# Attention and two feed-forward layers on one core: three instead of two scores ahead of the first value product of each half head

## The chip, the cores and the metric

The kernel runs on one core of a Trainium2 chip. The metric is the device time of one execution in microseconds (us); the median of several executions is compared.

## The reference, cut to what matters

Inputs are q, k, v of shape (2, 8, 768, 64) in fp32, a projection of 64 x 6, and the weights of two feed-forward layers. 16 heads of 768 tokens are worked on.

```python
q_bits = (q @ proj) > 0                      # 6 bits per token, likewise k_bits
mask = bucket(q_bits)[:, None] == bucket(k_bits)[None, :]
scores = where(mask, q @ k.T / 8, -1e9)
attn = exp(scores - max(scores)); attn = attn / (sum(attn) + 1e-9)
x = attn @ v                                 # per head, heads side by side: (1536, 512)
h = maximum(maximum(x @ w1, x @ w2), x @ w3) # 512 -> 768
y = h @ w_out                                # 768 -> 512
out = elu(y @ w_in) @ w_out2                 # 512 -> 2048 -> 512
```

## The kernel before, in words

**Precision.** Each fp32 operand of TensorE is split in a high and a low part of type fp32r, and a product is three matmuls (high x high, high x low, low x high). The mask is worked into the scores' matmuls as further rows of the operands, so one score is two matmuls (L621, L622).

**Slots.** Attention is a software pipeline over slots, one for each head, with some ahead of the first and behind the last (`all_slots`, L102; slots 4 to 11 are a loop of two turns with four slots each). Every engine runs its own list of work for a slot, ordered by hand and tied to the others by counting semaphores. A slot has 12 steps (`STEPS`), and `LAG` is 6: a half is 6 steps. In the slot of head h, TensorE does

- the 12 scores of head h (`scores`, L612), one a step: a tile of 128 keys by 384 queries; steps 0 to 5 are the first half of the queries, 6 to 11 the second. They go in turn to three PSUM banks (`RING` is 3), so score n waits until ScalarE has taken the exponentials of score n - 3 (`exp_done`, L618);
- 12 maxima of head h+1 (`maxima`, L597; L609), in the steps that `MAX_AT` (L65) sets: numbers 0 and 1 in step 0, 2 in step 1, 3 and 4 in step 2, 5 in step 3, 6 in step 4, 7 and 8 in step 5, 9 and 10 in step 6, 11 in step 7. They alternate between two PSUM banks, and maximum n waits until VectorE has reduced maximum n - 2 (`mx_read`, L607);
- 12 value products (`weigh`, L625; L636 to L638), six steps behind the scores: in steps 0 to 5 those of the second half of head h-1, in steps 6 to 11 those of the first half of head h. Six of them add up in one bank, `pv_ps`, there being only this one; the sixth is followed by L645, which signals `pv_ready`. The first of each six waits (`o_read`, L631) until ScalarE has copied the bank away;
- in odd slots transposes of q and k (L580) in steps 0 and 6, in even slots hash projections (L592 to L594) in steps 3 and 6. The last of these is in slot 12; slots 13 to 15 have none, and slot 15, the last head, has no maxima either;
- in step 8 the turn: the transpose of the row maxima (L667), which waits for `max_done` (L666), and a column sum (L672).

ScalarE in each step takes two exponentials of a score, `probs` (L378) and `p_hi` (L379). In steps 0 and 6 it first copies the finished `pv_ps` away, x (L356) and inv (L357) (`outcome`, L349). It also rounds v (`v_hi`, L387) behind the exponentials of step 0, and has work in steps 1, 3, 4 and 7 (L365, L418, L412).

VectorE reduces the maxima (L492). Between the reductions of maxima 2 and 3 it makes `v_lo` (L479), after maximum 11 the row maxima (L496). POOL makes `p_lo` (L335), one for each step, and one xl for each slot from 3 on (L341). SP moves operands.

**Order on TensorE** (`emit`, L648). In step 0 or 6 it is: the score of that step, the maxima, transposes or projections, the score of the next step, and then the first value product of the new half. In step 1 or 7: maxima, value product. In step 2 or 8: score, maxima, value product.

Behind attention TensorE goes through the feed-forward layers (`three`, L703, and L1050 to L1054).

Of the kernel before, what the change touches and what calls it, by code (L numbers as in the profile page):

```python
# [58 lines left out]
LAG = T  # L59
# [58 lines left out]
def wait(eng, sem, count):  # L118

    if not isinstance(count, int) or count > 0:  # L120
        eng.wait_ge(sem, count)


def attention(nc, q, k, v, proj, w1, w2, w3, xh, xl, raw, wh, wl, banks, w_loaded, w_split, w_ready, f_ready):
    ctx = ExitStack()
    with ctx:  # L126
# [436 lines left out]
        def _(pe):  # L563
            pe.wait_ge(consts, 3)

            def transposes(s, x, n):

                src = q_raw if x == "q" else k_raw
                par = (s.off + 3) // 2 % 2
                if n == 1:  # L570
                    pe.wait_ge(q_in[par], s.count(8, 56 - 16 * par))

                    wait(pe, bits_done, s.count(1, 3))
                else:
                    pe.wait_ge(k_in[par], s.count(8, 56 - 16 * par))
                    if s.off > FIRST_SLOT:
                        pe.wait_ge(lo_done, s.count(1, 4))
                out = turned[x, s.off == FIRST_SLOT]
                for t in range(T):
                    last = pe.transpose(out[:, t // TH, (t % TH) * P:(t % TH + 1) * P],  # L580
                                        src[:, par, t, :, :].rearrange("p a d -> p (a d)"), ident[:])
                last.then_inc(t_ready, 1)

            def project(s, x, n):


                pe.wait_ge(lo_done, s.count(1, 2 + n if s.off == FIRST_SLOT + 1 else 4))
                if s.off == FIRST_SLOT + 1:
                    pe.wait_ge(proj_split, 2)
                x_bank = misc[:, n - 1, 0:HALF]  # L590
                for c in range(2):
                    pe.matmul(x_bank, proj_hi[:, c, :], lo[x][:, c, :], start=(c == 0), stop=False)  # L592
                    pe.matmul(x_bank, proj_lo[:, c, :], hi[x][:, c, :], start=False, stop=False)
                    last = pe.matmul(x_bank, proj_hi[:, c, :], hi[x][:, c, :], start=False, stop=(c == 1))  # L594
                last.then_inc(hash_ready, 1)

            def maxima(s, n):  # L597

                m = s.off + 1
                if n == 0:  # L600

                    pe.wait_ge(spread1[m % 2], s.count(SPREAD1 / 2, SPREAD1 * (1.5 if m % 2 == 0 else 1)))
                    if m == 0:
                        pe.wait_ge(consts, 11)
                    wait(pe, mrow_done, s.count(1, 1))

                wait(pe, mx_read, s.count(STEPS, STEPS + n - 1))  # L607
                t, half = n // 2, (n % 2) * HALF
                pe.matmul(mx_ps[n % 2][:, 0:HALF], operands[m % GROUP][0:96, Q1, t * P:(t + 1) * P],  # L609
                          operands[m % GROUP][0:96, K1, half:half + HALF], start=True, stop=True).then_inc(mx_ready, 1)  # L610

            def scores(s, step):  # L612
                head = operands[s.off % GROUP]
                if step == 0:
                    pe.wait_ge(spread2[s.off % 2], s.count(SPREAD2 / 2, SPREAD2 / (1 if s.off % 2 == 0 else 2)))
                    pe.wait_ge(mrow_done, s.count(1, 1))

                wait(pe, exp_done, s.count(STEPS, step - RING + 1))  # L618
                t, half = step % T, step // T * HALF
                out = st_ps[step % RING][:, 0:HALF]  # L620
                pe.matmul(out, head[:, K1, t * P:(t + 1) * P], head[:, Q1, half:half + HALF], start=True, stop=False)  # L621
                pe.matmul(out, head[:, K2, t * P:(t + 1) * P], head[:, Q2, half:half + HALF], start=False, stop=True  # L622
                          ).then_inc(st_ready, 1)

            def weigh(s, step):  # L625

                h = s.off - (1 if step < LAG else 0)
                kt, at = step % T, (step - LAG) % STEPS
                if kt == 0:

                    wait(pe, o_read, s.count(4, -2 if step < LAG else 0))  # L631
                    if step == LAG:
                        pe.wait_ge(vl_done, s.count(1, 1))
                pe.wait_ge(pl_done, s.count(STEPS, step - LAG + 1))
                out, kept = pv_ps[:, 0:HALF], (STEPS * s.off + step - LAG) % KEPT
                pe.matmul(out, v_hi[:, h % 2, kt, :], p_hi[:, kept, :], start=(kt == 0), stop=False)  # L636
                pe.matmul(out, v_hi[:, h % 2, kt, :], p_lo[:, kept, :], start=False, stop=False)  # L637
                pe.matmul(pv_ps[0:D, 0:HALF], v_lo[:, h % 2, kt, :], p_hi[:, kept, :], start=False, stop=False  # L638
                          ).then_inc(pv_step, 1)
                if kt == T - 1:  # L640
                    if step > LAG:
                        pe.wait_ge(total_done, s.count(2, 2))
                        pe.wait_ge(empty_done, s.count(1, 1))
                    half = at // T * HALF
                    pe.matmul(out, total[:, h % 2, :], empty[:, h % 2, half:half + HALF], start=False, stop=True  # L645
                              ).then_inc(pv_ready, 1)

            def emit(s):  # L648
                for step in range(STEPS):
                    if s.has_st and step % LAG != 1:  # L650
                        scores(s, step)
                    if s.has_max:
                        for n in range(MAX_BEFORE[step], MAX_BEFORE[step + 1]):
                            maxima(s, n)
                    for i, x in enumerate("qk"):
                        if s.has_tp and step == TP_AT[i]:
                            transposes(s, x, i + 1)
                        if s.has_hash and step == HASH_AT[i]:
                            project(s, x, i + 1)
                    if s.has_st and step % LAG == 0:  # L660

                        scores(s, step + 1)
                    if s.has_half1 if step < LAG else s.has_half0:
                        weigh(s, step)
                    if step == TURN_AT and s.has_max:
                        pe.wait_ge(max_done, s.count(1, 2))  # L666
                        pe.transpose(mt_all, row_max[:, (s.off + 1) % 2, :], ident[:]).then_inc(mt_ready, 1)  # L667
                    if step == TURN_AT and s.has_st:
                        pe.wait_ge(vsum_done, s.count(1, 1))
                        if s.off == 0:  # L670
                            pe.wait_ge(consts, 15)
                        pe.matmul(sum_all, ones[:], val_sum[:], start=True, stop=True).then_inc(sum_ready, 1)  # L672
                if s.off == HEADS:


                    pe.wait_ge(w_ready, 1)
                    pe.wait_ge(xl_done, HEADS // B)
                    pe.wait_ge(exp_done, HEADS * STEPS)
                    for u, x in EARLY:
                        if (u, x) == (1, 0):  # L680
                            pe.wait_ge(w_ready, 2)
                            pe.wait_ge(mrow_done, HEADS)
                            pe.wait_ge(total_done, 2 * HEADS)
                        expert(pe, banks, wh, wl, xh, xl, u, x, f_ready)

            all_slots(pe, emit)


# [36 lines left out]
def expert(pe, banks, wh, wl, xh, xl, u, x, f_ready):  # L725

    m, c = UNIT_ORDER[u]
    pairs = []
    for t in range(KD):
        w = slice(x * DM + t * P, x * DM + (t + 1) * P)  # L730
        pairs.append(((wh[:, m % 2, w], wl[:, m % 2, w]), (x_tokens(xh, t, c), x_tokens(xl, t, c))))
    three(pe, banks[:, EXPERTS * (u % 2) + x, :], pairs).then_inc(f_ready, 1)
# [376 lines left out]
```

## Time and profile before

| | |
|---|---|
| three runs | 751.24, 752.99, 754.25 us; median 752.99 |
| the profiled execution, its own time | 751.45 us |
| its span, first to last instruction | 749.7 us |
| mean granted TensorE clock | 0.984 of 2.4 GHz |
| TensorE matmul busy | 719.0 us, 96% |
| VectorE, ScalarE, POOL busy | 379.8, 420.2, 366.5 us (51, 56, 49%) |

PE is TensorE's matmul row, PEld its weight load, DVE is VectorE, ACT ScalarE, POOL GpSimd. L-numbers are lines of the kernel. In a timeline a row has start, duration, engine, line, operation, output<-inputs, shape and count, and in brackets the idle time of the engine just before and what ended it. Matmuls overlap in their rows, since the shown duration has the way through the array in it; their rate is read from the starts. Attention takes about the first 287 us of the span.

### The profile page before, as it was taken

The numbers are of one execution on the slowest core, as the hardware profiler recorded it, in microseconds if no ns is written. First come the engines' busy times: TensorE is split into PE (matmuls) and PEld (weight loads), VectorE is DVE, ScalarE is ACT, GpSimd is POOL, SyncE is SP. The second block draws the span as 40 slices with busy tenths as digits, with TensorE's granted clock in tenths as the row PEclk, the third lists the DMA queues.
The fourth block names the chain that finished last, engine by engine and source line by source line (L and its number), as shares of the span: only waits on it lengthen the run. The fifth ranks groups of instructions, "written<-read, shape, count | busy, mean of one in ns | idle before, by whom it ended". The sixth has DMA issues, their size and how long they took to land.

```text
span 749.7 us, 10429 instructions
## 1 busy us (share of the span) xinstructions
PE 719.0 (96%) x3440; PEld 615.9 (82%) x3440; DVE 379.8 (51%) x612; ACT 420.2 (56%) x818; POOL 366.5 (49%) x332
## 2 busy tenths in 40 slices
PE   4699999999999989999999999999999999999998
PEld 3489999999999877788888888878888888888886
DVE  3677988889888854322222221144334343444333
ACT  1288989999898983222221121255556555555553
POOL 5077888888888883011110011154444545444452
PEclk9599999999999999999999999999999999999999
DMA  6766364563626100211000001033335332343331
GB/s 133 167 145 149 85 137 99 133 144 81 144 62 142 49 1 0 85 43 42 23 1 20 22 21 43 29 113 104 94 96 156 89 109 86 110 143 100 97 99 56
DMA packets 79629, 64.70 MB, mean 86 GB/s; under 512 B 29152, under 2 KB 68832, under 8 KB 79584
## 3 DMA queue, kind: packets, MB, share of 16 engines
q1 hardware_dynamic: 79584, 64.12, 33.6%
q8 instruction: 25, 0.41, 0.2%
q14 instruction: 20, 0.16, 0.1%
HBM read 40.91 MB, written 3.15 MB: 59 GB/s over the span
## 4 chain that ended last, share of the span: by engine, by line
PE 59%; DVE 0%; ACT 0%; issue 0%
PE banks L707 14%; PE banks L708 14%; PE banks L709 14%; PE banks L1050 6%; PE banks L1054 6%; PE banks L1051 6%; DVE g_sb L993 0%; DVE g_sb L989 0%; DVE out_sb L963 0%; ACT gh L948 0%; ACT neg L943 0%
## 5 line engine op out<-in xcount | busy, mean ns | idle before, releaser
L860 POOL TENSOR_TENSOR wl<-raw,wh 128x512 fp32r<-128x512 f32 (+2 forms) x104 | 143.4, 1398 | 301.7 <-ACT wh L876 301.7
L335 POOL TENSOR_TENSOR p_lo<-probs,p_hi 128x384 fp32r<-128x384 f32 x192 | 196.4, 1041 | 64.0 <-ACT p_hi L379 63.2
L707 PE MATMUL banks<-xh,wh 128*128 128x512 f32 x408 | 158.9, 390 | 0.5 <-PEq L126 0.5
L708 PE MATMUL banks<-xl,wh 128*128 128x512 f32 x408 | 158.7, 389 | 0.0
L709 PE MATMUL banks<-xh,wl 128*128 128x512 f32 x408 | 158.7, 389 | 0.0
L492 DVE TENSOR_REDUCE half_max<-banks 128x1 f32<-128x384 f32 x192 | 99.7, 547 | 28.2 <-PE banks L609 27.4
L378 ACT ACTIVATE probs<-banks 128x384 f32<-128x384 f32 x192 | 95.1, 495 | 23.2 <-PE banks L622 19.1
L379 ACT ACTIVATE p_hi<-banks 128x384 fp32r<-128x384 f32 x192 | 95.2, 496 | 0.0
L989 DVE TENSOR_SCALAR g_sb<-banks 128x512 f32<-128x512 f32 x48 | 33.2, 692 | 119.8 <-ACT neg L943 119.8
L707 PEld LDWEIGHTS banks<-xh,wh 128*128 128x128 f32 x408 | 76.6, 188 | 17.1 <-issue 0.9
L709 PEld LDWEIGHTS banks<-xh,wl 128*128 128x128 f32 x408 | 76.6, 188 | 15.9
L708 PEld LDWEIGHTS banks<-xl,wh 128*128 128x128 f32 x408 | 76.6, 188 | 15.7
L1050 PE MATMUL banks<-wh,gh 128*128 128x512 f32 x192 | 74.9, 390 | 0.2 <-ACT gh L948 0.2
L1054 PE MATMUL banks<-wh,gl 128*128 128x512 f32 x192 | 74.9, 390 | 0.0
L1051 PE MATMUL banks<-wl,gh 128*128 128x512 f32 x192 | 74.7, 389 | 0.0
L636 PE MATMUL banks<-p_hi,v_hi 128*128 128x384 f32 x192 | 67.0, 349 | 8.0 <-ACT inv L357 7.7
L943 ACT ACTIVATE neg<-banks 128x512 f32<-128x512 f32 x48 | 28.7, 598 | 68.1 <-PE banks L709 68.1
L876 ACT ACTIVATE wh<-raw 128x512 fp32r<-128x512 f32 (+2 forms) x104 | 64.7, 665 | 2.6 <-PE banks L1054 0.3
L638 PE MATMUL banks<-p_hi,v_lo 128*64 128x384 f32 x192 | 65.1, 339 | 0.0
L637 PE MATMUL banks<-p_lo,v_hi 128*128 128x384 f32 x192 | 64.4, 335 | 0.0
L922 ACT ACTIVATE hh<-e 128x512 fp32r<-128x512 f32 x18 | 11.4, 632 | 92.4 <-DVE e L973 92.4
L948 ACT ACTIVATE gh<-g_sb 128x512 fp32r<-128x512 f32 x48 | 30.4, 633 | 40.8 <-DVE g_sb L993 40.8
(108 smaller groups left out, 1175.9 us busy)
## 6 DMA issues: line engine op xcount, KB each, us to landing
operands<-wh SPq DMA_DIRECT2D x36, 384.0 KB, 6.9
raw<-in_moe_w_in SPq DMA_DIRECT2D x48, 256.0 KB, 2.7
raw<-in_moe_w_out SPq DMA_DIRECT2D x48, 256.0 KB, 2.8
wl<-wh SPq DMA_DIRECT2D x12, 384.0 KB, 5.8
raw<-in_moe_w SPq DMA_DIRECT2D x18, 256.0 KB, 3.8
q_raw<-in_q SPq DMA_DIRECT2D x16, 192.0 KB, 3.6
k_raw<-in_k SPq DMA_DIRECT2D x16, 192.0 KB, 3.8
v_raw<-in_v SPq DMA_DIRECT2D x16, 192.0 KB, 2.4
```

The lines of the kernel that those rows point to most:

```text
L335: pool.tensor_tensor(p_lo[:, at, :], probs[:, step % RING, :], p_hi[:, at, :].bitcast(FP32), ALU.subtract).then_inc(pl_done, 1)
L378: act.activation(probs[:, step % RING, :], scores, ACT.Exp, scale=SCALE)
L379: act.activation(p_hi[:, (STEPS * s.off + step) % KEPT, :], scores, ACT.Exp, scale=SCALE).then_inc(exp_done, 1)
L492: dve.tensor_reduce(half_max[:, m % 2, n // 2, n % 2:n % 2 + 1], mx_ps[n % 2][:, 0:HALF], AX.X, ALU.max).then_inc(mx_read, 1)
L636: pe.matmul(out, v_hi[:, h % 2, kt, :], p_hi[:, kept, :], start=(kt == 0), stop=False)
L707: pe.matmul(out, sh, mh, start=first, stop=False)
L708: pe.matmul(out, sh, ml, start=False, stop=False)
L709: last = pe.matmul(out, sl, mh, start=False, stop=final)
L860: pool.tensor_tensor(wl[:, j, at:at + cols], raw[:, j, at:at + cols], wh[:, j, at:at + cols].bitcast(FP32), ALU.subtract).then_inc(w_ready, 1)
L1050: pe.matmul(acc[t], gh[:, n % 2, cols], w2h, start=(k == 0), stop=False)
L1051: pe.matmul(acc[t], gh[:, n % 2, cols], w2l, start=False, stop=False)
L1054: last = pe.matmul(acc[t], gl[:, n % 2, cols], w2h, start=False, stop=(k == M2 - 1))
```

## The change

On entering each half, TensorE issues the score of step 2 (or 8) right behind that of step 1 (or 7), ahead of the first value product of the half, and not any more at the start of step 2 (or 8). The matmuls, their operands, banks and waits stay the same.

```diff
             def emit(s):
                 for step in range(STEPS):
-                    if s.has_st and step % LAG != 1:
+                    if s.has_st and step % LAG not in (1, 2):
                         scores(s, step)
                     if s.has_max:
                         for n in range(MAX_BEFORE[step], MAX_BEFORE[step + 1]):
                             maxima(s, n)
...
                     if s.has_st and step % LAG == 0:

                         scores(s, step + 1)
+                        scores(s, step + 2)
                     if s.has_half1 if step < LAG else s.has_half0:
                         weigh(s, step)
```

## Rows read from the trace of the kernel before

**Rows 1.** The page, part 1: busy us, share of the span, instructions.

```profile
PE 719.0 (96%) x3440; PEld 615.9 (82%) x3440; DVE 379.8 (51%) x612; ACT 420.2 (56%) x818; POOL 366.5 (49%) x332
```

**Rows 2.** Waits on PE; idle time before L636: us, times, longest.

```profile
PE banks L636 <- ACT inv L357: 7.7, 13, 2.1
...
  ACT inv L357: 20.3, 30
```

**Rows 3.** Timeline, first half of an even slot: PE, its loads, DVE.

```profile
158.54 0.34 PE L622 MATMUL banks<-wl 128*128 128x384 f32 x1
...
159.19 0.44 PE L636 MATMUL banks<-p_hi,v_hi 128*128 128x384 f32 x1 [0.31 <-ACT inv L357]
...
159.82 0.34 PE L609 MATMUL banks<-operands 96*128 96x384 f32 x1
...
160.20 0.56 DVE L492 TENSOR_REDUCE half_max<-banks 128x1 f32<-128x384 f32 x1 [0.34 <-PE banks L609]
...
160.67 0.79 DVE L479 TENSOR_TENSOR v_lo<-v_raw,v_hi 128x384 fp32r<-128x384 f32 x1
...
161.38 1.01 DVE L492 TENSOR_REDUCE half_max<-banks 128x1 f32<-128x384 f32 x2
...
161.75 0.19 PEld L622 LDWEIGHTS banks<-wl 128*128 128x128 f32 x1
...
161.98 0.19 PEld L609 LDWEIGHTS banks<-operands 96*128 96x128 f32 x1
162.10 0.34 PE L609 MATMUL banks<-operands 96*128 96x384 f32 x1
```

**Rows 4.** Timeline, first half of an odd slot: PE, DVE, POOL.

```profile
144.88 0.34 PE L609 MATMUL banks<-wl 96*128 96x384 f32 x1
...
145.26 0.56 DVE L492 TENSOR_REDUCE half_max<-banks 128x1 f32<-128x384 f32 x1 [0.56 <-PE banks L609]
...
145.73 0.59 DVE L479 TENSOR_TENSOR v_lo<-v_raw,v_hi 128x384 fp32r<-128x384 f32 x1
...
146.19 1.02 POOL L335 TENSOR_TENSOR p_lo<-probs,p_hi 128x384 fp32r<-128x384 f32 x1 [0.28 <-ACT p_hi L379]
...
146.32 1.02 DVE L492 TENSOR_REDUCE half_max<-banks 128x1 f32<-128x384 f32 x2
```

**Rows 5.** Timeline, second half of the same odd slot: PE, DVE, PEld.

```profile
151.94 0.33 PE L622 MATMUL banks<-operands 128*128 128x384 f32 x1
152.30 0.44 PE L636 MATMUL banks<-p_hi,v_hi 128*128 128x384 f32 x1
152.58 0.34 PE L637 MATMUL banks<-p_lo,v_hi 128*128 128x384 f32 x1
...
152.93 0.34 PE L609 MATMUL banks<-wl 96*128 96x384 f32 x1
...
153.91 0.18 DVE L496 TENSOR_REDUCE row_max<-half_max 128x12 f32<-128x24 f32 x1
...
154.35 0.14 PEld L667 LDWEIGHTS banks<-ident,row_max 128*128 128x128 f32 x1
```

**Rows 6.** Timeline, slot 0: v_lo on DVE and p_lo on POOL.

```profile
37.19 1.36 DVE L479 TENSOR_TENSOR v_lo<-v_raw,v_hi 128x384 fp32r<-128x384 f32 x1
...
37.13 1.00 POOL L335 TENSOR_TENSOR p_lo<-probs,p_hi 128x384 fp32r<-128x384 f32 x1 [0.28 <-ACT p_hi L379]
```

**Rows 7.** Timeline of slot 13, and busy times of one stretch of slot 15.

```profile
244.92 0.44 PE L636 MATMUL banks<-p_hi,v_hi 128*128 128x384 f32 x1 [0.68 <-ACT inv L357]
...
240.10 0.49 ACT L378 ACTIVATE probs<-banks 128x384 f32<-128x384 f32 x1 [0.29 <-PE banks L622]
...
271.00:276.00 5.00, 2.25 (x10) 1.25 (x10) 0.50 (x1) 4.90 (x11) 3.91 (x4) 1.00 0.00 0
```

**Rows 8.** Busy times of 277 to 281 us: PE, PEld, DVE, ACT, POOL, then granted clock.

```profile
277.00:281.00 4.00, 4.00 (x16) 3.81 (x16) 2.22 (x4) 2.05 (x6) 2.99 (x4) 0.57 0.00 0
```

## The prediction

> **What bounds the kernel now.** I read the page first: TensorE is busy 96% of the span [rows 1], so time can only come from its few pauses or from doing less work, and the change does the same matmuls in another order. The page's chain of waits runs through the feed-forward part, which the diff does not touch; the diff acts in attention. So the waits came next: the value product's first matmul (L636) waits for the second evacuation of its single accumulator (L357) 7.7 us in all on the matmul row, and the idle time before it, with the weight load's row counted too, is 20.3 us at 30 places [rows 2]. These overlap, so neither is the price. I took the price from starts in the timeline. Back-to-back matmuls of 384 columns start 0.175 us apart (152.58 to 152.93 holds two) [rows 5].
>
> Entry of an even slot, where nothing else stands between the scores: last score matmul at 158.54, value product at 159.19, so 0.65 - 0.175 = 0.475 us lost [rows 3]. Entry of the second half of an odd slot, where transposes fill part of it: 151.94 to 152.30, 0.185 us lost, and 0.28 instead of 0.175 to the next matmul, another 0.10 [rows 5]. In the steady part (slots 1 to 12) there are six of each kind. Odd slots at step 0 and even slots at step 6 have transposes or projections there and lose nothing. In slots 13 to 15 there are six more, of which the one at 244.92 (0.68 idle) stands here [rows 7].
>
> **The change, part by part.** One score, two matmuls, 2 x 0.175 = 0.35 us, moves from behind the second value product to ahead of the first. It has no transfer, and passes no work of SP's or POOL's queue. It does pass the maxima of step 1 (maximum 2 in the first half, 11 in the second) and two value products. Its own wait is for the previous exponentials (step 5's for step 8). The outcome's two copies follow that exponential on ScalarE, so the score's wait is over about 1 us before that of the value product queued behind it: price 0.
>
> What matters is what becomes close together. Between maximum 2 and maxima 3 to 5 there stood this score; maximum n may start only when VectorE has read n-2.
>
> *A. First half of even slots, six.* The value product cannot start before the copy, so maximum 2 stays at 159.82. VectorE reads it from 160.20, then makes v_lo (160.67, 0.79 us), then reads maxima 3 and 4 from 161.38, the first by about 161.93 (0.56 us). Maximum 5's weight load starts at 161.98, though its predecessor's started at 161.75 and loads follow 0.175 apart: it is already late by 0.05, waiting for that read [rows 3]. So this chain (copy, value product, maximum 2, v_lo, maximum 3, maximum 5) is closed before the change; filling the pause at its start cannot bring maximum 5 at 162.10 forward. The freed 0.35 us turns up as a wait at maxima 4 and 5. Gain 0; bounds -0.35 and +0.1 each (-2.1, +0.6).
>
> *B. First half of odd slots, six.* No pause there, so value product and maximum 2 go 0.35 later: 144.88 becomes 145.23. VectorE reads maximum 2 0.38 us after its start for 0.56 us [rows 4]; with the 0.05 that a release takes in [rows 3], maximum 4's load may start 0.99 after maximum 2 and its matmul 0.12 later (161.98 to 162.10), 1.11 in all. TensorE would be there after 0.88 (one maximum, three products, one maximum: five of 0.175). That adds 0.23. v_lo starts at 146.08, and maximum 3 is then read in time for maximum 5. Cost 0.22 x 6 = +1.3 us; bounds 0 and the whole score, 0.35 x 6 = +2.1.
>
> *C. Second half of odd slots, six.* The 0.185 + 0.10 of pause goes, since 0.35 more work stands ahead: 0.28 x 6 = -1.7 us; bounds -2.1 and 0.
>
> *D. The turn of the row maxima, slots 0 to 14.* In the second half the score leaves the stretch between maximum 11 (152.93) and the turn's transpose (L667), whose load is at 154.35 [rows 5]. Row maxima are ready at 153.91 + 0.18 = 154.09, 1.16 after maximum 11; released at 1.21, the matmul starts at 1.33. Without the score TensorE is there after 0.175 + 6 x 0.175 = 1.23. A new wait of 0.10 x 15 = +1.5 us; bounds 0 and 0.2 x 15 = +3.0.
>
> *E. Slots 13 to 15.* The first-half entries of 13 and 14 are closed by the chain of A, but step 3's score still comes 0.12 earlier, and ScalarE was idle 0.29 waiting for it [rows 7], so the next copy comes 0.12 earlier too. Their second halves have no v_lo and long pauses: 0.35 each. Slot 15 has no maxima, but ScalarE is back to back there (busy 4.90 of 5.00 us [rows 7]); only the score left behind its second entry gains, 0.35. Sum -(0.12 + 0.35) x 2 - 0.35 = -1.3 us; bounds -2.1 and 0.
>
> *F. Slot 0.* It enters no half with the accumulator in use. Maximum 2 is later, but v_lo ends when POOL is done anyway [rows 6]: 0; bounds 0 and +0.5.
>
> Sum: 0 + 1.3 - 1.7 + 1.5 - 1.3 + 0 = -0.2 us. The profiled execution took 751.45, so its like would take 751.25; it lay 1.54 below the median of the runs, 752.99, against which I state the forecast: **752.8 us**.
>
> Here the trace and the notes can be weighed. Both [rows 3] and [rows 5] show the weight load starting no earlier than the release, and the matmul some 0.1 behind its usual place. The Trainium skill (TensorE: Matmul & The Clock Gate, Architectural detail) says that TensorE's queue can pull weight loads ahead of matmuls in flight. If that reached past a semaphore wait, B would cost about 0.11 and D nothing, and the sum would be about -2.4. The rows do not show it, so the sum keeps the 0.1.
>
> **Rivals.** *Full gain:* the maxima's reads are quick enough after all, and every pause shrinks by up to 0.35: 6 x 0.28 + 12 x 0.35 = 5.9, so 747.1 us. For it: the pauses are there. Against it: the late load of maximum 5 in [rows 3]. Chance 0.10.
>
> *Slower, v_lo behind POOL:* in slot 0 v_lo started at 37.19, 0.06 after a p_lo of POOL, and took 1.36 instead of 0.59, ending 0.42 after POOL did [rows 4, 6]. In odd slots v_lo moves to 146.08, and the next p_lo starts at 146.19 [rows 4]. The margin is 0.11. If v_lo comes second it ends at 147.21 + 0.42 = 147.63, maximum 3 is read by 148.1, and maximum 5's matmul starts near 148.3 instead of 147.20: +1.1 in place of 0.22, 6 x 0.88 = +5.3, so 758.1 us. It decides where v_lo slips by more than 0.11 us. Chance 0.12. The Trainium skill (SBUF — State Buffer, Who interferes with whom) has a rule for it: a VectorE instruction with two inputs in SBUF contends with a GpSimd instruction that reads SBUF, and the first gets the shared port for its whole length. By that rule, the trace agrees, with the 1.36.
>
> *The clock:* from 277 to 281 us the granted clock averages 0.57, so mostly 1.2 instead of 2.4 GHz, after a stretch with TensorE busy 2.25 of 5.00 us [rows 8, 7]. A score now stands inside that pause. If the drop goes, some ten matmuls save 0.14 each (384 columns at 1.2 GHz are 0.32 us, against 0.175): 1.4 us, 751.4 us. Chance 0.08; still no change by the bound below.
>
> **How the numbers follow.** About 0.5%, 3.8 us, is what a measurement can tell from no change: below 749.2 faster, above 756.8 slower. My sum keeps 0.70. Its bounds are not independent; with B and D at their low ends it is -3.0 (750.0), with both high +2.1 (755.1), and runs spread 1.5 around their median. The range 749.5 to 756.0 holds this case and the clock's; full gain and the POOL case are left out. Faster: 0.10 plus a little for A opening, 0.12. Slower: 0.12 plus 0.01, 0.13. Same: 0.75.
>
> **What would show it.** In the changed trace the pause ahead of L636 should be below 0.2 at even entries and gone in odd second halves; L609 should gain waits for L492, about 0.2 at maximum 4 in every first half, and maximum 5 in even slots should again start 2.28 after maximum 2; L667 should wait about 0.1 for L496. An even slot's first half, from value product to maximum 5, keeps its 2.91 us. Wrong if the wait at L636 shrinks and no wait at L609 takes its place (full gain), or if v_lo in odd slots takes over 1 us (slower).

## The result and the profile after

The changed kernel took 756.54 us (median of five runs, 756.35 to 757.35). The kernel before, beside it on the same chip, took 752.92 (five runs, 751.24 to 754.25). The ratio is 1.0065, with a 95% interval of 1.0049 to 1.0080: **slower by about 0.65%**, just outside the range of 749.5 to 756.0. The ratio is not the quotient of these two medians, which is 1.0048: the median of before and three of its five runs lie in a cluster near 753, and against the 751.6 that later groups of runs of the same kernel gave (below) it is 1.0066. The profiled execution of the changed kernel is one of 756.84 us with a span of 755.0, 5.39 and 5.3 above those of before, so the two traces hold the whole difference and some more.

The page after (its part 1, and from part 5 the group of the value product's first matmul):

```profile
PE 724.0 (96%) x3440; PEld 614.0 (81%) x3440; DVE 381.2 (50%) x612; ACT 419.1 (56%) x818; POOL 367.5 (49%) x332
...
L636 PE MATMUL banks<-p_hi,v_hi 128*128 128x384 f32 x192 | 66.8, 348 | 2.3 <-ACT inv L357 2.2
```

The instruction counts are those of [rows 1]. TensorE's busy time has grown by 5.0 us with the same work, so it can't tell where time was lost: a matmul row grows when the clock is lower. The waits in attention, from 50 to 290 us of the kernel after, say more (engine, line, what it waited for: us, times, longest):

```profile
ACT probs L378 <- PE banks L622: 21.4, 22, 2.1
PEld banks L609 <- DVE half_max L492: 11.6, 27, 1.0
...
PEld banks L636 <- ACT inv L357: 5.1, 10, 1.7
PE banks L609 <- DVE half_max L492: 3.8, 8, 0.7
...
PEld banks L668 <- DVE row_max L496: 2.7, 14, 0.2
...
PE banks L636 <- ACT inv L357: 2.2, 4, 1.4
```

The wait that the change aims at did shrink, from 7.7 us at 13 places [rows 2] to 2.2 at 4. In its place the maxima (L609) wait for VectorE, 3.8 us on the matmul row and 11.6 on that of the loads (the two overlap). And ScalarE waits 21.4 us for scores; in the same window of the kernel before it was 12.6.

To find where, I took the starts of L645, the last matmul of each half, and their distances. Each row stands for the halves of that kind; in us:

| half | before | after | difference in all |
|---|---|---|---|
| odd slots 1, 3, 7, 9, 11, first half | 7.71 to 7.75 | 7.88 to 7.90 | +0.83 |
| slot 5, first half | 7.70 | 8.76 | +1.06 |
| odd slots, second half, six | 7.16 to 7.32 | 6.98 to 6.99 | -1.61 |
| even slots 2 and 4, first half | 8.71, 8.72 | 8.72, 8.72 | 0.0 |
| **even slots 6, 8, 10, 12, first half** | 8.62 to 8.65 | 9.94 to 9.97 | **+5.26** |
| even slots, second half, six | 7.28 to 7.34 | 7.33 to 7.39 | +0.27 |
| slots 13, 14, first halves | 7.52, 7.66 | 7.51, 7.66 | 0.0 |
| slots 13, 14, second halves; 15, first | 7.23, 7.37, 6.23 | 6.87, 7.01, 5.87 | -1.08 |
| slot 15, second half | 10.76 | 11.67 | +0.91 |

The first L645 comes 0.26 earlier than before and the last one 5.38 later, at 292.40 against 287.02. Nearly all of the loss is in four halves. Slot 8's shows how, in the timeline of the kernel after (it answers to [rows 3]; rows of TensorE, its loads, VectorE, ScalarE and POOL):

```profile
160.35 1.01 POOL L335 TENSOR_TENSOR p_lo<-probs,p_hi 128x384 fp32r<-128x384 f32 x1
...
160.41 1.38 DVE L535 TENSOR_TENSOR x<-x,inv 128x384 f32<-128x384 f32 x1
...
160.91 0.44 PE L636 MATMUL banks<-p_hi,v_hi 128*128 128x384 f32 x1
...
161.70 1.64 DVE L492 TENSOR_REDUCE half_max<-banks 128x1 f32<-128x384 f32 x3
...
162.30 0.44 PE L609 MATMUL banks<-operands 96*128 96x384 f32 x1 [0.60 <-DVE half_max L492]
...
163.07 2.29 POOL L335 TENSOR_TENSOR p_lo<-probs,p_hi 128x384 fp32r<-128x384 f32 x2 [0.31 <-ACT p_hi L379]
...
163.25 1.24 DVE L479 TENSOR_TENSOR v_lo<-v_raw,v_hi 128x384 fp32r<-128x384 f32 x1
...
164.75 0.49 ACT L378 ACTIVATE probs<-banks 128x384 f32<-128x384 f32 x1 [1.00 <-PE banks L622]
...
165.02 0.44 PE L609 MATMUL banks<-operands 96*128 96x384 f32 x1 [0.31 <-DVE half_max L492]
```

The same place in the kernel before, rows that the prediction did not use:

```profile
158.38 1.41 POOL L335 TENSOR_TENSOR p_lo<-probs,p_hi 128x384 fp32r<-128x384 f32 x1
...
158.39 0.54 DVE L535 TENSOR_TENSOR x<-x,inv 128x384 f32<-128x384 f32 x1
```

Read L535 first. It is VectorE's division of a finished head (`divide`, x times inv), the last thing in its list for a slot, from slot 2 on, and so the one of an odd slot stands ahead of maximum 0 of the even slot. The description of the kernel before leaves it out. Both its inputs are in SBUF. Before, it started 0.01 us after a p_lo of POOL and took 0.54, while that p_lo took 1.41 in place of 1.01. After, it started 0.06 behind a p_lo and took 1.38, ending 0.43 after POOL. So of the two, one keeps its time and the other ends late, and the change has turned round who comes first. The 0.84 lost there make the reductions of maxima 0 to 2 late (161.70), maximum 2 waits 0.60 on the matmul row, v_lo starts at 163.25, 0.18 behind a p_lo (163.07), and takes 1.24; before it came 0.64 behind one (160.03) and took 0.79 [rows 3], maximum 5 comes 2.72 after maximum 2 instead of 2.28, and ScalarE, without scores for 1.00 us, hands the delay on.

The starts of the division and of that p_lo in four of the five pairs of the steady part, both kernels:

| end of slot | before: division, p_lo | after: division, p_lo | division took, before, after |
|---|---|---|---|
| 3 | 96.44, 96.45 | 96.38, 96.38 | 0.56, 0.56 |
| 5 | 127.42, 127.45 | 128.20, 128.02 | 0.56, 1.25 |
| 7 | 158.39, 158.38 | 160.41, 160.35 | 0.54, 1.38 |
| 9 | 189.33, 189.34 | 192.57, 192.52 | 0.54, 1.38 |

The end of slot 11 is like that of 9 (224.80, 1.37). Slot 4, which follows the one tie that was still won, keeps its 8.72, and slot 2 has no division ahead of it. A lost tie is not dear everywhere: at the ends of the even slots 4 to 10 the division came second in the kernel before as well (1.23 to 1.26), and run 2 below, which frees it there, leaves the odd first halves at 7.69 to 7.85, against 7.70 to 7.75.

Why it tips, at the end of slot 7: both engines are back to back up to this point, on chains that start at different matmuls. VectorE's starts at the reduction of maximum 11, 5.08 us ahead of the division before and 5.05 after (153.31 to 158.39, 155.36 to 160.41). POOL's starts at the p_lo of step 8, three p_lo ahead of the one in the tie (155.46 before, 157.42 after). The change issues the score of step 8 earlier and thereby maximum 11 later against it: from the reduction to that p_lo it was 2.15 us, and is now 2.06. These 0.09 are more than the margin.

The stretch that answers to [rows 4], the first half of odd slot 7 after:

```profile
147.08 0.34 PE L609 MATMUL banks<-wl 96*128 96x384 f32 x1
...
147.45 0.56 DVE L492 TENSOR_REDUCE half_max<-banks 128x1 f32<-128x384 f32 x1 [0.92 <-PE banks L609]
147.93 0.55 DVE L479 TENSOR_TENSOR v_lo<-v_raw,v_hi 128x384 fp32r<-128x384 f32 x1
...
148.04 1.31 POOL L335 TENSOR_TENSOR p_lo<-probs,p_hi 128x384 fp32r<-128x384 f32 x1 [0.29 <-ACT p_hi L379]
...
148.06 0.19 PEld L609 LDWEIGHTS banks<-wl 96*128 96x128 f32 x1 [0.27 <-DVE half_max L492]
```

v_lo stays 0.11 ahead of POOL and takes 0.55 us; in four of the other odd slots it is 0.11 to 0.19 ahead, with the same 0.55. Its second half (it answers to [rows 5]):

```profile
154.99 0.34 PE L609 MATMUL banks<-wl 96*128 96x384 f32 x1
...
155.95 0.18 DVE L496 TENSOR_REDUCE row_max<-half_max 128x12 f32<-128x24 f32 x1
...
156.03 0.34 PE L638 MATMUL banks<-p_hi,v_lo 128*64 128x384 f32 x1
...
156.18 0.14 PEld L668 LDWEIGHTS banks<-ident,row_max 128*128 128x128 f32 x1 [0.19 <-DVE row_max L496]
...
156.20 0.31 PE L668 MATMUL banks<-ident,row_max 128*128 128x128 f32 x1
```

The load of the turn waits 0.19, but the matmul starts 0.17 after the one before it: no pause.

### The profile page after: what moved, and what is told of

It reads as the page before. It is cut to its first block, busy times and chain, and to the rows that moved or that the text cites. A ratio compares the mean times of both kernels' runs of the same rounds, so it can differ in the third digit from the quotient of the medians.

```text
span 755.0 us, 10429 instructions
## 1 busy us (share of the span) xinstructions
PE 724.0 (96%) x3440; PEld 614.0 (81%) x3440; DVE 381.2 (50%) x612; ACT 419.1 (56%) x818; POOL 367.5 (49%) x332
## 4 chain that ended last, share of the span: by engine, by line
PE 59%; DVE 0%; ACT 0%; issue 0%
PE banks L708 14%; PE banks L709 14%; PE banks L710 14%; PE banks L1051 6%; PE banks L1055 6%; PE banks L1052 6%; DVE g_sb L994 0%; DVE g_sb L990 0%; DVE out_sb L964 0%; ACT gh L949 0%; ACT neg L944 0%
## 5 line engine op out<-in xcount | busy, mean ns | idle before, releaser
L636 PE MATMUL banks<-p_hi,v_hi 128*128 128x384 f32 x192 | 66.8, 348 | 2.3 <-ACT inv L357 2.2
L621 PE MATMUL banks<-operands 128*128 128x384 f32 x144 | 51.8, 360 | 2.3 <-ACT p_hi L379 2.3
```

## The experiments

My theory: the loss is the tie at L535, some 1.3 us for each of the four that are lost, with little else changed. The rival: the even first halves lose through the entry itself (three scores ahead, maximum 2 late, v_lo late), whatever the division does. Each kernel is compared with the kernel before of its own group of runs, whose medians were 751.55 (runs 1 to 4), 751.74 (5, 8, 9 and 10), 751.57 (6, 11 and 12) and 751.60 (7). The ratios are estimated from the single runs and need not be the quotients of the medians. In the expectations the runs go by labels: e1 to e5 are runs 1 to 5, e6, e7 and e8 are 8, 9 and 10, e9 is 6, e10 and e11 are 11 and 12, and e12 is 7.

**1. The change, with the division moved.** The tie goes, the change stays.

```diff
@@ VectorE, emit
+                    if n == 2 and s.has_split:
+                        divide(Slot(s.off - 1, s.g))
@@ end of the slot
-                if s.has_unit:
-                    divide(s)
```

> Three scores ahead as in the change, but VectorE's division (L535, two SBUF inputs) is issued behind the second reduction of the next slot instead of ahead of the first. Theory 'lost port': in slots 6, 8, 10 and 12 of the changed kernel the division starts 0.05 to 0.2 us after a p_lo of POOL, takes 1.25 to 1.38 instead of 0.55 us, and delays maxima 2 to 5; with it out of the way these four first halves fall from 9.95 to about 8.7 us, so about 756.5 - 5.2 = 751.3 us. Rival 'chain of maxima': the tighter order of maxima 2 to 5 alone makes the 9.95, the division is only late with them; then 756.5 stays.

Measured: 751.14 us (749.18 to 752.61, ten runs), 0.9991 of before [0.9974, 1.0007]. The four halves are back at 8.63 to 8.66, those of slots 2 and 4 stay at 8.71 and 8.74. The tile x on VectorE, and the division in slot 8:

```profile
L535 DVE TENSOR_TENSOR x<-x,inv x16: 545/549/1371, 81.8 to 291.2; 128x384 f32<-128x384 f32 x16
...
158.97 0.55 DVE L535 TENSOR_TENSOR x<-x,inv 128x384 f32<-128x384 f32 x1
```

Its median over all slots is 0.549 us; in the kernel before it was 1.013, with those ahead of odd slots at 1.23 to 1.33. The odd halves keep what the change did to them (7.89 to 8.00, and 6.98 to 7.00). The rival falls: the entry with three scores is still there, and with the division out of the way maximum 2 comes 1.81 after maximum 0 (157.37 and 159.18), as in the kernel before (158.01 and 159.82), and v_lo takes its 0.79.

**2. The kernel before, with the division moved**, the control.

> The kernel before with the same move of the division. Theory 'lost port': before the change the division takes 0.55 us in even slots, so nothing is to be had there: 752.9 us, within 1.5. Rival 'the move is a gain of its own': it falls by about as much as e1 does against the changed kernel, to 748.

Measured: 752.21 (751.38 to 754.57), 1.0008 [0.9991, 1.0026]. Moving the division brings nothing by itself, so what run 1 won back is the change's own loss.

**3. The third score ahead in first halves only.** Then the score of step 8 stays behind maximum 11, and the tie should stay as it was.

```diff
-                    if s.has_st and step % LAG not in (1, 2):
+                    if s.has_st and step % LAG != 1 and step != 2:
...
-                        scores(s, step + 2)
+                        if step == 0:
+                            scores(s, step + 2)
```

> Only the first halves (step 0) get the third score. Theory 'lost port': maximum 11 and the row maxima stay where they were against ScalarE, so the division keeps its tie with POOL, and only the new wait of odd first halves is paid, 6 x 0.17 = 1 us, less about 0.1 each in slots 13 and 14: 753.8 us. Rival 'first halves are the cause': 756 or more.

Measured: 753.44 (752.09 to 756.11), 1.0027 [1.0008, 1.0046]. In the trace the divisions take 0.54 to 0.55 at all even entries, and even first halves 8.63 to 8.73: no tie is lost. Odd first halves take 7.88 to 7.94, which is the cost of step B, here 1.1 us for the six. The last half of this trace takes 7.85 instead of 4.92 at a granted clock of 0.74 and 0.83, so its profiled time is no measure of the edit.

**4. The third score ahead in second halves only.** The tie should be lost, with the first halves as before.

```diff
+                    if s.has_st and step % LAG != 1 and step != 8:
...
+                        if step == 6:
+                            scores(s, step + 2)
```

> Only the second halves (step 6) get the third score. By halves of the two traces, odd second halves gain 0.17 to 0.33 (six, 1.7), slots 13 to 15 0.36 each (1.1), even ones lose 0.06 (0.4): -2.4 without any lost port, 750.5 us. Theory 'lost port': in odd slots the value product, and with it maximum 11 and the division, comes about 0.17 later against ScalarE and POOL, and the division's tie is lost: four to six first halves of even slots at +1.3, so 755.7 to 758.3 us. Rival 'the loss needs both halves' (the late value product of the first half): 750.5.

Measured: 752.06 (750.15 to 753.05), 1.0000 [0.9982, 1.0018]: far less than I expected. The trace has the ties lost at the entries of slots 6, 8 and 12 (9.93 to 9.94 for the half) and won at slot 10 (8.69), by 0.02 us:

```profile
160.16 1.42 DVE L535 TENSOR_TENSOR x<-x,inv 128x384 f32<-128x384 f32 x1
...
192.15 0.55 DVE L535 TENSOR_TENSOR x<-x,inv 128x384 f32<-128x384 f32 x1
...
192.17 1.40 POOL L335 TENSOR_TENSOR p_lo<-probs,p_hi 128x384 fp32r<-128x384 f32 x1
```

So the mechanism is where I put it, and its size in the median was missed. In this trace the three lost ties cost 3.9 us and slot 5's first half 1.05, even second halves 0.3; odd second halves give back 1.6, the second halves of 13 and 14 0.6, and slot 15's second half 1.9, since it takes 8.86 instead of 10.76 with the clock at 2.4 GHz throughout (below). The sum is +1.1, near the +1.2 between the last L645 of the two kernels (288.22 against 287.02). A part of the price was thus hidden by the clock. How many ties the other nine runs lost can't be seen in their times; with one tie won by 0.02 us, and two of the three lost ones at starts that differ by 0.001 us, it may differ from run to run.

**5 and 6. The tie turned over in the kernel before, with nothing else changed.** Run 5 puts a memset of 128 x 64 ahead of the division in slots 3, 5, 7, 9 and 11, run 6 one of 128 x 384.

```diff
+        spare = sb("spare", [P, 64])        # run 6: [P, HALF]
...
+                    if s.odd and s.off < HEADS - 3:
+                        dve.memset(spare[:], 0.0)
                     divide(s)
```

> The kernel before with one small memset (64 columns, own tile) ahead of VectorE's division at the end of slots 3, 5, 7, 9 and 11. Theory 'lost tie': before, the division and a p_lo of POOL start within 0.03 us of each other there and the division goes first; 0.1 us later it goes second, takes 1.3 to 1.4 instead of 0.55 us, and the first halves of slots 4, 6, 8, 10 and 12 grow from about 8.65 to 9.95 us: 5 x 1.3 = 6.5, so 758 us (four lost: 757). Rival 'a delay of 0.1 us on VectorE costs 0.1 us': 752 us, halves of 8.7.

> e5 with a memset of 384 instead of 64 columns, since the small one moved the division by only 0.02 us and one tie of five was lost (that half 9.28 instead of 8.65 us). Now the division starts 0.3 to 0.4 us later, behind a p_lo that has begun. Theory 'lost tie': it takes 1.2 to 1.4 us in all five places and the first halves of slots 4, 6, 8, 10 and 12 cost 0.6 to 1.3 us more each: 751.7 + 3 to 6.5 = 754.7 to 758.2 us. Rival 'the delay alone': VectorE idles 0.34 us ahead of maximum 2 there, so 0 to 0.1 each, 752 us.

Measured: run 5 752.81 (749.93 to 754.29), 1.0003 [0.9989, 1.0017]; run 6 754.14 (752.54 to 754.62), 1.0034 [1.0022, 1.0045]. Both missed, since neither did what it was made for. In run 5 one division of five came second (156.90, against a p_lo at 156.85; 1.36 us, and the half takes 9.28); the other four started 0.04 to 0.06 behind their p_lo and yet took 0.48 to 0.50, with the p_lo at 1.41. In run 6 too it was one of five, at the end of slot 7 (160.34, against 159.97; 1.04 us, and the half takes 9.28). The other four are like this one, at the end of slot 3:

```profile
97.91 1.75 POOL L336 TENSOR_TENSOR p_lo<-probs,p_hi 128x384 fp32r<-128x384 f32 x1
...
98.00 0.38 DVE L524 MEMSET spare<- 128x384 f32 x1
98.30 0.49 DVE L538 TENSOR_TENSOR x<-x,inv 128x384 f32<-128x384 f32 x1
```

The division starts 0.39 after the p_lo and yet takes 0.49, and the p_lo takes 1.75 instead of 1.01. It looks as if the memset itself had come first, and the division behind it kept POOL out; that is not shown. A delay that was meant to be neutral was not. But these four are a control for the next run: the memset kept VectorE for 0.38 us without a division coming second, and the even first halves behind them grew by 0.01 to 0.10 alone. Of the 2.4 us that run 6 lies above its group's kernel before, its halves hold 1.1 (0.6 of it the lost tie); its first L645 comes 1.45 later than in the trace of before, ahead of the first memset.

**7. The same with a reduction**, an operation with one input, of which [rows 4] show that it runs beside a p_lo at its usual 0.5 us.

```diff
+        spare = sb("spare", [P, 1])
...
+                    if s.odd and s.off < HEADS - 3:
+                        dve.tensor_reduce(spare[:], ident[:], AX.X, ALU.max)
                     divide(s)
```

> As e5 and e9, but with a reduction of 128 columns to one in the place of the memset. In e9 POOL's p_lo grew where the division stayed at 0.49 us, so the memset itself had gone first and kept POOL out; a reduction has one input. It should move the division by 0.15 to 0.2 us and leave POOL to begin. Theory 'lost tie': the division takes 1.2 to 1.4 us in all five places, and with v_lo still on time each such half costs about 0.65 us more, as the one in e5 and the one in e9: 5 x 0.65 = 3.3, so 751.6 + 3.3 = 754.9 us; 758 where v_lo is late too. Rival 'the delay alone': 752 us.

Measured: **757.19 (756.57 to 758.00), 1.0080 [1.0052, 1.0108]**. VectorE and POOL, end of slot 7:

```profile
160.02 0.27 DVE L524 TENSOR_REDUCE spare<-ident 128x1 f32<-128x128 f32 x1
160.21 1.25 DVE L538 TENSOR_TENSOR x<-x,inv 128x384 f32<-128x384 f32 x1
...
160.05 1.00 POOL L336 TENSOR_TENSOR p_lo<-probs,p_hi 128x384 fp32r<-128x384 f32 x1
...
162.94 0.55 DVE L480 TENSOR_TENSOR v_lo<-v_raw,v_hi 128x384 fp32r<-128x384 f32 x1
```

All five divisions take 1.24 to 1.26. Five reductions of 0.2 us in the kernel before thus cost as much as the whole change, and it isn't the delay: run 6 delays VectorE by more. The price is smaller by the tie: the five even first halves take 9.24 to 9.30, +0.6 each, with v_lo not second as well (162.94, 0.55). So a lost tie costs 0.6 to 0.7 with v_lo first, and 1.3 in the change, where v_lo loses too. These five make 3.1 of the 5.0 us between its profiled execution (756.60) and the median of before; slot 5's first half adds 0.4, and slots 15 and 16 add 1.4, 1.5 less in one half and 2.9 more in the last, where the low clock fell in this trace. I can't say whether the reductions brought that last part with them.

**8 to 12. A version that beats both.** With the division moved, what is left to win is the closed chain of step A: copy, value product, maximum 2, v_lo, maximum 3, maximum 5. Run 8 makes v_lo later too, behind the reduction of maximum 5; run 9 also issues maximum 2 right behind the third score. Run 10 is the control for both, the kernel before with division and v_lo late.

```diff
-                    if n == MAX_BEFORE[V_AT + 2] and s.has_st:
+                    if n == MAX_BEFORE[V_AT + 4] and s.has_st:
... run 9 as well, TensorE's emit:
-                            maxima(s, n)
+                            if not (s.has_st and n == 2):
+                                maxima(s, n)
...
+                    if s.has_st and s.has_max and step == 0:
+                        maxima(s, 2)
```

> e1 with v_lo made behind the reduction of maximum 5 instead of ahead of that of maximum 3. Step A of the prediction says that the chain value product, maximum 2, v_lo, maximum 3, maximum 5 holds the first half of even slots at 8.7 us; with v_lo out of it the freed 0.35 us less the wait of maximum 4 (0.1 to 0.2) can show: 8.35 to 8.55, six times, so e1's 751.1 falls to 749 to 750. Rival 'the half is bounded otherwise' (the matmuls themselves, or ScalarE): 751.1.

> e6 with maximum 2 of each slot issued behind the third score, ahead of the first value product. The wait of maximum 4 for the reading of maximum 2 (0.22 us in odd and even first halves, steps A and B) goes too: odd first halves from 7.9 to about 7.7, even ones by a further 0.1 to 0.2, in all 2 us under e6: 747.5 us. Rival 'maximum 4 waits for something else': as e6.

> The kernel before with division and v_lo as late as in e6, two scores ahead. Control: v_lo does not bind by more than 0.05 us a slot there, so 751 to 752 us. If it falls as far as e6, the third score has no part in the gain.

Measured: run 8 750.52 (750.26 to 751.57), 0.9983 [0.9970, 0.9995]; run 9 749.47 (749.10 to 749.79, four runs), 0.9957 [0.9940, 0.9974]; the control 751.71 (749.69 to 754.82), 0.9996 [0.9978, 1.0014]. The even first halves fall to 8.43 to 8.60 and then to 8.2 to 8.4, while odd first halves take 7.98 to 8.04, 0.3 more than before. The late v_lo does that and not the third score, since the control has 7.99 to 8.02 as well. Both runs stay short of what was expected of them (749 to 750, and 747.5), run 9 above all because its odd first halves did not fall to 7.7.

Run 11 takes the third score in second halves alone, with the division moved (the edits of runs 4 and 1 together), the half of the change that has a pause to fill:

> e4 with the division out of the way. Steps C, D and E alone by the halves of the traces: -1.7 + 0.4 - 1.1 = -2.4 us against before, so 749.3 us, and about 2 under e4 (three lost ties at about 1.25, against a clock drop that e4's profile did not have). Rival 'e4's gain is eaten elsewhere': 752.

Measured: 750.04 (748.59 to 751.76), 0.9981 [0.9968, 0.9995]. Odd first halves keep 7.69 to 7.80, odd second halves have 6.98 to 7.03. Run 12 puts each part only where the halves showed a gain:

```diff
+    wide = property(lambda s: not s.odd or s.off >= HEADS - 3)
...
+                    if n == MAX_BEFORE[V_AT + (4 if s.wide else 2)] and s.has_st:
...
+                    if n == 2 and s.has_split:
+                        divide(Slot(s.off - 1, s.g))
...
+                        if step == 6 or s.wide:
+                            scores(s, step + 2)
+                    if s.has_st and s.has_max and s.wide and step == 0:
+                        maxima(s, 2)
```

> A version meant to beat both: e7, but in odd slots up to 11 the first half keeps two scores, maximum 2 in step 1 and v_lo ahead of maximum 3 (there the third score only cost: 7.71 us before, 7.89 in the changed kernel, 8.0 in e7). Against e7 six odd first halves fall by 0.3: 749.5 - 1.8 = 747.7 us. Rival: odd halves stay at 8.0 because of the moved division, and 749.5 stays.

Measured: **747.36 (746.87 to 749.09, six runs), 0.9952 [0.9938, 0.9965]**, faster than both kernels. Entry of an even slot in its timeline (TensorE and VectorE):

```profile
157.93 0.44 PE L610 MATMUL banks<-operands 96*128 96x384 f32 x1
158.21 0.34 PE L637 MATMUL banks<-p_hi,v_hi 128*128 128x384 f32 x1
...
158.26 0.54 DVE L536 TENSOR_TENSOR x<-x,inv 128x384 f32<-128x384 f32 x1
...
161.34 1.06 DVE L480 TENSOR_TENSOR v_lo<-v_raw,v_hi 128x384 fp32r<-128x384 f32 x1
```

The value product follows maximum 2 without a wait for the copy, the division has its 0.54, and v_lo may take 1.06 where nothing waits for it. Even first halves are 8.38 to 8.41, slot 2's 8.20. Not every tie is won in this version either: in slot 1 maxima 0 and 1 wait for the bits of the operands, v_lo then starts 0.15 behind a p_lo and takes 1.27, and the half takes 9.16 instead of 7.70, though the L645 that it starts from comes 0.88 earlier.

## Why the prediction was wrong

**The step that failed** is step A, "0; bounds -0.35 and +0.1 each". Its chain began at the value product and took VectorE to be free when maximum 0 comes; what VectorE does just before, the division that ends the odd slot, has no place in the prediction. It was in the trace of before: L535 with 0.54 against a p_lo of 1.41, and elsewhere with 1.23 to 1.33. In four of six even first halves the step was off by +1.3 us, 5.3 in all, about as much as the change's whole loss. In slot 4, where the tie was won, and in slot 2, which has no division ahead, A's 0 is right to 0.01; with the division moved (run 1) it is right to 0.02 in all six.

**The rival had the mechanism, at another instruction.** *Slower, v_lo behind POOL* gave 758.1 for a two-input VectorE instruction that comes second to a p_lo, 0.88 a slot in six odd slots, at a chance of 0.12. In five odd slots v_lo kept a lead of 0.11 to 0.19 and its 0.55 us, so the rival's sign, over 1 us there, never showed. The lock closed one slot on, at the division, whose margin was 0.01 instead of 0.11. That the sum, +5.3, agrees with the +5.4 of the traces is chance. The rule on the shared port from the Trainium skill, which the prediction named for v_lo (SBUF — State Buffer, Who interferes with whom), fits the division as well: by it, an instruction with two inputs in SBUF contends with a reading GpSimd instruction, and the trace agrees, with 1.38 against 0.54. I applied it to one of VectorE's instructions of that kind and not to all.

**Where it was right.** *B:* maximum 4's load starts 0.98 after maximum 2, forecast 0.99, and odd first halves cost 0.15 to 0.19 each, forecast 0.22; five of six. *C with D:* odd second halves gain 1.60 in all, forecast 1.7 - 6 x 0.10 = 1.1; in part because D was smaller. *D* is the term that was mis-sized: even second halves lose 0.03 to 0.07, not 0.10, since the matmul started 0.02 behind its load, not 0.12. Of the two loads in the rows above that wait out a release, the one ahead of a matmul of 384 columns gives 0.1 away (148.06 to about 148.17), the one ahead of the short matmul of the turn does not. *E:* second halves of 13 and 14 gain 0.36 each, forecast 0.35 less D's 0.10. Their first halves gain nothing; the 0.12 each were not there. Slot 15 gains its 0.36 in the first half, not in the second as forecast (10.76 before and in run 1, at the same place of the clock's drop). In all 1.1, forecast 1.1. *F:* the first L645 comes 0.26 earlier, not 0. All of it without the four ties, slot 5 and slot 15 is 5.4 - 5.3 - 0.9 - 0.9 = -1.7 us, 1.5 better than the -0.2 of the sum. The prediction's own bound for slower, 756.8, was too wide as well: 756.54 lies below it, and yet the interval of the ratio is clear of 1.

**Slot 5's first half** lost 0.9 more than its like. Its maxima 0 and 1 waited for the bits of the operands (until 112.27), maximum 2 came at 114.60 instead of 113.96, and v_lo started at 115.45, behind a p_lo at 114.96, and took 0.93: here the forecast rival did happen, once. In the waits it is one row:

```profile
PE banks L609 <- DMA operands<-bits: 0.3, 1, 0.3
```

Why that transfer landed late I did not find; it was late in run 4 as well, with the half at 8.75.

**The clock** rival went against its sign. Busy times of PE, PEld, DVE, ACT and POOL and then the granted clock, kernel after (it answers to [rows 8]), and under it run 4:

```profile
276.00:280.00 4.00, 1.73 (x6) 0.96 (x6) 0.33 (x1) 3.93 (x10) 3.27 (x4) 0.88 0.00 0
280.00:284.00 4.00, 4.00 (x14) 3.34 (x14) 0.00 (x0) 2.86 (x7) 3.23 (x4) 0.50 0.02 4
284.00:288.00 4.00, 3.81 (x17) 3.32 (x16) 2.62 (x4) 2.50 (x6) 2.46 (x3) 0.76 0.00 0
```

```profile
276.00:280.00 4.00, 2.47 (x11) 1.74 (x12) 0.00 (x0) 3.91 (x9) 3.13 (x4) 1.00 0.01 4
280.00:284.00 4.00, 3.63 (x22) 3.17 (x20) 3.15 (x4) 3.82 (x11) 4.00 (x4) 1.00 0.00 0
```

The drop to 1.2 GHz (0.50) did not go but lasted about twice as long; it follows a stretch with TensorE busy 1.73 of 4.00 us, and slot 15's second half takes 0.91 longer. In run 4, with 2.47 of 4.00 there, the clock stays at 2.4 GHz and the half takes 8.86. Low activity alone did not decide it either: in run 7 TensorE was busy 1.32 of 4.00 us from 276 to 280 and the clock stayed at 1.00, and it fell to 0.57 only from 288 to 292. So the drop falls differently from trace to trace, with 1 to 3 us at stake. The runs of the kernel before lie in clusters near 749.8, 751.5, 753.0 and 754.4, and the traces point to a second source for these: the first L645 stands at 49.56 in the kernel before, at 47.91 in run 5, 51.02 in run 2 and 51.01 in run 6, which are the same kernel up to there. Steps of 1.5 us thus arise ahead of all that is argued about here, and the distances between the L645 are a better measure of an edit than one execution's time. What makes the steps is not shown.

## What to carry to other kernels

Before moving work on the engine that is the bound, list for the two engines that hold each other up (here VectorE and POOL) every pair of instructions that run at the same time, with the margin by which one comes first; a margin of 0.01 us in the trace of before is a cost waiting to be paid, not a state to build on. Look in particular at what an engine does at the end of the stretch before the one that you edit. A VectorE instruction with two SBUF inputs is best put where POOL is known to be idle or where nothing waits for it: here moving the division by two reductions made the change harmless, and placing each part only where the trace had a pause gave 0.5%.

## What the hardware showed that I had not expected

A two-input VectorE instruction of 128 x 384 in fp32 takes 0.54 to 0.56 us if it is first, and if it is second it ends about 0.42 after POOL's; POOL's takes 1.0 alone and 1.38 to 1.42 where the division came first. Near a tie the recorded starts do not decide it: the division won at 0.01 behind (158.39 against 158.38) and lost at 0.05 and 0.06 behind, but in run 4 it also lost twice where it was recorded 0.001 ahead (160.16, 1.42 us). A reduction of 0.2 us ahead of it is enough to turn five of five (run 7). A memset on VectorE, which reads nothing, was not neutral: beside it p_lo took 1.75 us, and a division that started 0.39 after that p_lo still took only 0.49. Whether the memset or the division held POOL up there is not settled.
